# A three-stage mixer kernel on one core: the first batch's loads, last unit, up projections and weight pieces put in another order

## The reference

```python
state = alpha[:, :, t, :, None] * state + einsum('bhd,bhe->bhde', k[:, :, t], v[:, :, t])
y[:, :, t] = einsum('bhd,bhde->bhe', q[:, :, t], state)      # 4 batches, 8 heads, 768 steps, 48 wide
...
h = x.transpose(0, 2, 1) @ U @ V                             # x = y, 768 x 384; rank 32
u = x + h.transpose(0, 2, 1)
x2 = u + maximum(u @ w_ch1, 0) @ w_ch2                       # 384 -> 1536 -> 384
...                                                          # second block on x2
```

## Time and profile before

| | |
|---|---|
| time, median of 3 runs | 664.71 us (663.87 to 665.14) |
| the profiled execution's own time | 663.96 us |
| its span (first to last instruction) | 662.2 us |
| PE busy | 648.3 us, 98% of the span |
| DVE, ACT, POOL busy | 320.2, 263.2, 255.5 us |
| granted TensorE clock, mean | 0.997 |

### The profile page before, as it was taken

How to read it: one execution, slowest core, us unless ns; L and a number is a source line. 1 busy time by engine, 2 the same in 40 slices (tenths; PEclk the granted TensorE clock), 3 DMA queues, 4 the chain that set the end, 5 groups by cost and what they waited for, 6 DMA issues and landing times.

```text
span 662.2 us, 15677 instructions
## 1 busy us (share of the span) xinstructions
PE 648.3 (98%) x6370; PEld 624.8 (94%) x6370; DVE 320.2 (48%) x542; ACT 263.2 (40%) x542; POOL 255.5 (39%) x250
## 2 busy tenths in 40 slices
PE   7889999999999999999999999999999999999998
PEld 4778999999999999999999999999999999999998
DVE  7956664255563255663242215765425543444522
ACT  5765544334544234444233334434324321432320
POOL 6777742133323133332112562347314531733220
PEclk9899999999999999999999999999999999999999
DMA  8674203006103015110015350220041023002101
GB/s 319 226 282 158 73 27 103 2 25 238 47 7 124 2 57 205 47 38 2 1 37 185 103 168 12 75 82 25 13 138 64 0 69 121 24 0 83 60 1 71
DMA packets 25018, 54.84 MB, mean 83 GB/s; under 512 B 2176, under 2 KB 16896, under 8 KB 24960
## 3 DMA queue, kind: packets, MB, share of 16 engines
q1 hardware_dynamic: 24960, 53.99, 23.6%
HBM read 44.55 MB, written 9.44 MB: 82 GB/s over the span
## 4 chain that ended last, share of the span: by engine, by line
PE 94%; DVE 2%; issue 2%; ACT 1%; POOL 0%; POOLq 0%; ACTq 0%
PE banks L764 23%; PE banks L794 22%; PE banks L1159 22%; PE banks L1231 6%; PE banks L1077 5%; PE banks L397 4%; PE banks L1134 2%; PE banks L458 2%; PE banks L526 2%; PE banks L518 2%; PE banks L1541 1%; PE banks L712 1%; PE banks L657 1%; DVE tokiL L247 1%; PE banks L717 1%
## 5 line engine op out<-in xcount | busy, mean ns | idle before, releaser
L778 DVE SCALAR_TENSOR_TENSOR hidL<-banks,hidH 128x384 fp32r<-128x384 f32 x96 | 53.4, 557 | 124.5 <-ACT hidH L774 124.1
L764 PE MATMUL banks<-uH,w1H 128*128 128x384 f32 x288 | 100.1, 347 | 0.0
L794 PE MATMUL banks<-hidH,w2H 128*128 128x384 f32 x288 | 96.6, 335 | 2.2 <-issue 1.4
L764 PE MATMUL banks<-uL,w1H 128*128 128x384 f32 x288 | 96.9, 337 | 0.5 <-POOL uL L749 0.5
L764 PE MATMUL banks<-uH,w1L 128*128 128x384 f32 x288 | 96.6, 335 | 0.0
L794 PE MATMUL banks<-hidH,w2L 128*128 128x384 f32 x288 | 96.5, 335 | 0.0
L794 PE MATMUL banks<-hidL,w2H 128*128 128x384 f32 x288 | 96.3, 334 | 0.0
L774 ACT ACTIVATE hidH<-banks 128x384 fp32r<-128x384 f32 x96 | 47.0, 489 | 87.9 <-PE banks L764 87.9
L1217 POOL TENSOR_TENSOR u2L<-x_res,u2H 128x384 fp32r<-128x384 f32 x24 | 24.4, 1017 | 95.9 <-ACT u2H L1211 95.9
L383 POOL TENSOR_TENSOR k_end<-qka_sb,tail 112x384 f32<-112x384 f32 x32 | 30.1, 940 | 73.8 <-DVE tail L346 70.4
L794 PEld LDWEIGHTS banks<-hidH,w2H 128*128 128x128 f32 x288 | 54.1, 188 | 3.4 <-issue 3.0
(11 more groups left out here) (131 smaller groups left out, 1405.7 us busy)
## 6 DMA issues: line engine op xcount, KB each, us to landing
qka_sb<-qka SPq DMA_DIRECT2D x29, 582.5 KB, 5.8
v_sb<-v_nat SPq DMA_DIRECT2D x32, 144.0 KB, 5.7
stage<-w SPq DMA_DIRECT2D x6, 768.0 KB, 4.5
x_dram<-u_t SPq DMA_DIRECT2D x8, 576.0 KB, 3.7
x_f<-x_dram SPq DMA_DIRECT2D x12, 384.0 KB, 4.2
x_res<-x_dram SPq DMA_DIRECT2D x8, 576.0 KB, 4.2
out_t<-stage SPq DMA_DIRECT2D x24, 192.0 KB, 1.9
stage<-tok_r_t SPq DMA_DIRECT2D x3, 768.0 KB, 4.6
```

The source lines that it names most:

```text
L764: last = nc.tensor.matmul(ps[:, 0:HALF], w[:, f, P * k:P * (k + 1)], x[half][:, k, :], start=(k == 0 and i == 0), stop=(k == DM_TILES - 1 ...
L778: nc.vector.scalar_tensor_tensor(hidL[s % 2][:], hid_ps[s % 2][:, 0:HALF], 0.0, hidH[s % 2][:].bitcast(F32), ALU.max, ALU.subtract).then_i ...
L794: last = nc.tensor.matmul(acc[m][:, 0:HALF], w[:, f, P * m:P * (m + 1)], x[s % 2][:], start=(f == 0 and i == 0), stop=(f == F_TILES - 1 an ...
```

## The change

All of it is in the first batch and in the slots of its MLP.

```diff
+        def load_alpha(sp, u):
+            sp.dma_start(qka_sb[u][:, 2 * HALF:ROW], qka[0, u, :, 2 * HALF:ROW]).then_inc(S[ALPHAS[u]], 16)
...
-                sp.dma_start(qka_sb[i][:, 2 * HALF:ROW], qka[b, u, :, 2 * HALF:ROW]
-                             ).then_inc(S[ALPHAS[u]], 16)
...
+        HI_TERMS, LO_TERM = (0, 1), (2,)
+
-        def hidden_products(pe, b, s, ks):
+        def hidden_products(pe, b, s, ks, terms=(0, 1, 2)):
...
-        EARLY_HI = (range(0, 0), range(0, 0), range(0, 1), range(1, 2), range(2, 3), range(3, 4), range(4, 7), range(7, 8))
+        EARLY_HI = (range(0, 0), range(0, 0), range(0, 1), range(1, 2), range(2, 3), range(3, 4), range(4, 6), range(6, 8))
...
-        AHEAD_LO, FIRST_LO = range(8, 10), range(10, 13)
+        FIRST_LO = range(8, 10)
...
@@ SP, first batch @@
             for u in range(2):
+                load_alpha(sp, u)
+            for u in range(2):
                 load_unit(sp, 0, u)
             load_v(sp, 0, 0)
+            load_alpha(sp, 2)
             load_unit(sp, 0, 2)
...
             sp.wait_ge(S["rel_done"], 5)
-            for u in range(6, UNITS):
-                load_unit(sp, 0, u)
-                load_v(sp, 0, u)
+            load_unit(sp, 0, 6)
+            load_v(sp, 0, 6)
+            sp.wait_ge(S["rel_done"], 6)
+            load_unit(sp, 0, 7)
+            load_v(sp, 0, 7)
             sp.wait_ge(S["tail_done"], 7)
             load_weight(sp, 1)
-            sp.wait_ge(S["rel_done"], UNITS)
+            sp.wait_ge(S["st_done"], 6)
             load_weight(sp, 2)
@@ PE, end of the first batch @@
                 pe_state(pe, 0, u + 1)
-                if u == UNITS - 2:
-                    first_g(pe, UNITS - 3).then_inc(S["early_g_ready"], 1)
                 pe_carried(pe, 0, u).then_inc(S["y_ready"], 1)
+            first_g(pe, UNITS - 3).then_inc(S["early_g_ready"], 1)
+            pe_values(pe, 0, UNITS - 1).then_inc(S["half_done"], 1)
+            pe_carried(pe, 0, UNITS - 1).then_inc(S["y_ready"], 1)
             pe.wait_ge(S["rel_done"], UNITS)
             lr_turn(pe, 0, 0, 0).then_inc(S["first_turned"], 1)
-            pe_values(pe, 0, UNITS - 1).then_inc(S["half_done"], 1)
-            pe_carried(pe, 0, UNITS - 1).then_inc(S["y_ready"], 1)
...
             lr_product(pe, 0, 0, 0)
+            pe.wait_ge(S["y_done"], UNITS)
+            lr_product(pe, 0, 0, 1)
             first_g(pe, UNITS - 2)
             first_g(pe, UNITS - 1).then_inc(S["g_ready"], 1)
             pe.wait_ge(S["x_t_done"], 1)
             lr_turn(pe, 0, 0, 2).then_inc(S["first_turned"], 1)
-            lr_product(pe, 0, 0, 1)
             pe.wait_ge(S["g_done"], 1)
             lr_product(pe, 0, 0, 2)
-            hidden_products(pe, 0, 0, range(DM_TILES - 1))
-            hidden_products(pe, 0, 1, range(DM_TILES - 1))
+            for s in range(BEGUN):
+                hidden_products(pe, 0, s, range(1))
+                hidden_products(pe, 0, s, range(1, 2), HI_TERMS)
+            for s in range(BEGUN):
+                hidden_products(pe, 0, s, range(1, 2), LO_TERM)
```

More of the change, by code:

```diff
@@ L984, in mlp_batch_pool @@
             if first_batch(b):
-                for i in AHEAD_LO:
-                    part_lo(pool, i)
                 pool.wait_ge(S["uL_done"], LR_HALF)
```

15 lines of the change are left out of this document (7 added, 8 removed).

## The result

The changed kernel takes **668.74 us** (median of 6 runs, 666.94 to 670.15); the kernel before, run beside it, 664.31 us (6 runs, 663.56 to 665.14). The ratio is 1.0065, with a 95% interval of 1.0047 to 1.0084. The prediction, 662.8 us with a range from 661.6 to 665.9 us, is wrong in its sign. The profiled execution has a span of 667.9 us against 662.2 us, and its mean granted clock is 0.99 instead of 0.997.

What follows compares the result with a forecast made beforehand. PE, busy 648.3 of 662.2 us, was taken as the bound, so only its idle time could change. Terms 0 - 0.96 - 0.87 + 2.31 - 0.81 - 1.56 = -1.89 us gave 662.8 us against the median, range 661.6 to 665.9.

Steps and rivals of the forecast that it cites:

- the race: Whether PE's program request, at about 29.9 us, goes ahead of the third weight load at 29.70 us; taken as won.
- First loads: At the start, second alpha ahead of first q and k: DVE's 0.48 us wait at most; taken as 0, -0.4 to +0.2.
- Unit 7's load held to rel_done 6: In unit 5's scores, PE's program fetch goes ahead of this load and DVE's mask wait goes: -0.96 us.
- Third weight load held to st_done 6: In unit 7's state products, the program request goes first and PE's stop ahead of 35.82 us goes: -0.87 us.
- Rival 1: The fetch stays behind the third weight load, so 0.2 of 1.83 us gain is left: 664.5 us, chance 0.18.
- rival 2: Fetches take their time whatever is loaded, so both PE stops in the first batch stay: 664.6 us, chance 0.12.
- The last unit ahead: End of first batch: last unit before gates and turns delays output copy on ACT and last gate products: +2.31 us.
- rival 3: Half clock after the turn, at the up projections, following PE idle time: 1.2 to 1.7 us more, 664.1 us, chance 0.16.
- Two up projections in a row: After the turn, high terms of both tiles ahead of block 1's low terms cut PE's idle time: -0.81 us.
- Weight pieces: Fewer POOL pieces ahead of the next batch's queries remove PE's 1.40 us wait in slot 2: -1.56 us.
- The cover that was named: Behind the next batch's first queries, 18 or more PE matmuls between piece groups; if it failed, 1.2 us once.

Runs made afterwards that it cites:

- the clean base: The kernel before with unit 7's loads held to rel_done 6 and the third weight load to y_ready 6: 663.52 us, ratio 0.9984.
- the mended one: The changed kernel with y_ready for the third weight load, ACT's pieces ahead of the turned copy and first loads in old order: 662.66 us, ratio 0.9981.

## Why the prediction was wrong

Four steps failed: the first loads, the race, the clock behind the turn, and the price of the pieces.

**"First loads", taken at 0 between -0.4 and +0.2: mis-sized.** The prediction saw DVE's wait for alpha and not what alpha stands in front of. It measured +1.79 us at the scan of 14.50 us. Its reason for nothing, that PE's restart at 21.10 us is held by a fetch whatever comes before, did not hold: that restart came at 22.95 us, 1.85 us later. How much of it reaches the end stays open: alone 1.8 us by the medians and 1.1 us by the ratio, with a stop of 2.45 us in the trace; on the clean base 0.4 us in the median and 2.5 us between the two traces.

**"Unit 7's load held to rel_done 6", -0.96: right in the main.** Measured -0.82 us at the mask, PE's stop down to 0.15 us. In the other kernels with this hold and without the late first loads, stops of up to 0.71 us remain, and the mask waits up to 0.41 us.

**"Third weight load held to st_done 6", -0.87: the choice of the likelier case failed.** The text had 29.70 us against about 29.9 us and took the race as won "because the load's first packet comes later than its issue". It was lost in the traces of all kernels that had it, by 0.1 to 0.4 us between issue and PE's restart. The reason given was true and did not help: the load's first packet came 0.8 us behind its issue, and the program packet comes 1.5 us behind a restart even with no load in its way. Rival 1 then counted a stop no longer than before; it was 1.71 us instead of 0.68 us, +0.8 us at that place. The load, held back, now starts 0.4 us ahead of the restart, so that the request waits for nearly all of it. The mechanism itself, a request that waits for a load, was right: a later signal removes the stop, and with it rival 2, by which no load would matter, is out.

**"The last unit ahead", +2.31: the size was right, what follows it was not.** At full clock the gates of units 6 and 7 came 2.0 us later against gates of unit 5 (39.97 - 34.65 = 5.32 us, before 40.07 - 36.07 = 4.00 us, and the 0.68 us of carried products that now stand ahead), and the chain through ACT was as described. But rival 3, half clock after the turn, had a chance of 0.16 and was seen in the profiled run of every kernel that had this order with its gaps unfilled, save the mended one, whose gaps (0.43, 0.89 and 0.38 us) were like those of the clean base. All six runs of the changed kernel have a mean clock of 0.99 or 0.992, three stretches or more. It costs 1.3 us for 6.8 us of half clock on the clean base, within the 1.2 to 1.7 us that rival 3 gave; in the changed kernel it lasted 10.2 us. There the stop of the lost race and the gap of the new order stand one behind the other. So the step that failed is the weight given to it, not its size.

**"Two up projections in a row", -0.81: nothing that can be told**; -0.17 us and -0.67 us at the turn behind slot 0.

**"Weight pieces", -1.56: right at its place, wrong behind it.** Slot 2's wait is gone to the hundredth. "I cost them at nothing" is the fourth failure: pieces that moved on stand in pairs beside DVE's scans, which stand still meanwhile, and about 1.2 us of the 1.6 lost by the end are lost there. The cover that was named, PE's matmuls between two groups, was counted against the pieces alone and not against a slower DVE.

At the ledger's places the misses are 3.6 us ahead of the turn (first loads 1.8, the race 1.7, the mask 0.1), 2.4 us in it (about 1.9 us of them the clock, an estimate from 1.3 us for 6.8 us of half clock), 0 at slot 2 and 1.6 us behind it: 7.6 us, from -1.9 to +5.7 us. That the stop brings half clock is shown by the kernels that differ in it alone: 10.2 us of it in the trace with the stop and none without, a mean clock of 1.00 in 2 of 12 runs and in 5 of 12. That the five parts together cost more than one by one is not shown. How much of the 10.2 us of half clock the late first loads account for was not separated.

## What to carry to other kernels

A load that is to be held behind an engine's request for its program needs a signal that comes clearly after the request; a signal near it makes the stop longer. Here 1.3 to 1.6 us behind the restart was enough and 0.1 us ahead of it was not; the line should lie near 0.7 us behind it (an estimate: 1.5 us from restart to program packet less 0.8 us from issue to first packet). Before a small transfer is put ahead of a large one, look at who waits for the large one; and before work goes to a second engine "in the shade", look at which instructions of the other engine it will slow in that place (here scans with both inputs in SBUF), and in how long a row. Short idle times of PE in like small matmuls are to be counted twice, once as idle time and once for the clock of the matmuls behind them.

## What the runs showed of the hardware

- A program packet of PE came near the end of the data load issued before PE's restart (129 data packets ahead of it from 31.4 to 35 us, 15 beside and behind it); with the load issued 1.57 us behind the restart it came before the load's first packet, 1.5 us behind the restart. PE went on 2.1 to 3.0 us behind the packet.
- A DVE scan with both inputs in SBUF takes 0.95 us alone and 2.6 to 2.8 us beside two POOL instructions of 0.99 us each; it ends 0.8 us behind them. The other way round, POOL's queries take 0.94 us alone and 1.50 us when a state scan began just ahead of them (16.63 and 16.79 us, the changed kernel).
- The granted clock fell to 0.50 for 3.4, 6.8 or 10.2 us after gaps of PE that sum to 1.3 to 3.0 us among small matmuls, in some runs of a kernel and not in others; in three traces also behind a single wait of 1.4 us ahead of 128x384 products (54.6 to 58.0 us in one), which in the profiled run of the kernel before did not happen.
- An alpha load put ahead of unit 0's q and k made these about 2 us later.
